# Attention with the new state ahead of the weighted values, and a last projection taken token tile by token tile

## What is computed

```python
# 1 gated linear attention, per batch and head, over time t
m_new = max(f + m, i); f_stab = exp(f + m - m_new); i_stab = exp(i - m_new)
C = f_stab * C + i_stab * outer(v, k);  n = f_stab * n + i_stab * k
y = sigmoid(o_gate) * (C @ q) / max(|n @ q|, 1)
# 2 MLP, 320 -> 2048 -> 320
h = x @ w_in;  x = maximum(0.01 * h, h) @ w_out
# 3 eight experts, 320 -> 1024 -> 320, weighted by P
P = exp(x @ w_gate), normed 8 times over rows and columns
out = sum over e of P[:, e] * (maximum(x @ w1[e], 0) @ w2[e])
```

## Time and profile before

| | us |
|---|---|
| median of 3 runs | 949.97 (949.3 to 950.03) |
| the profiled execution, its own time | 952.44 |
| its span, first to last instruction | 950.7 |
| TensorE busy in the span | 937.6 |
| mean granted TensorE clock | 0.996 |

### The profile page before, as it was taken

How to read it: one execution, slowest core, us unless ns; L and a number is a source line. 1 busy time by engine, 2 the same in 40 slices (tenths; PEclk the granted TensorE clock), 3 DMA queues, 4 the chain that set the end, 5 groups by cost and what they waited for, 6 DMA issues and landing times.

```text
span 950.7 us, 16706 instructions
## 1 busy us (share of the span) xinstructions
PE 937.6 (99%) x6529; PEld 892.7 (94%) x6529; DVE 648.5 (68%) x1066; ACT 360.6 (38%) x659; POOL 440.9 (46%) x501
## 2 busy tenths in 40 slices
PE   8999999999999999999999999999999999999998
PEld 5889888888789999999999999999999999999998
DVE  6577555457777899876766666676666666766664
ACT  5666443344454333333323332342343233233221
POOL 4364042046688656475742653473265257336000
PEclk9899999999999999999999999999999999999999
DMA  7961222002011111111211121021112101110000
GB/s 131 208 119 22 61 62 67 1 1 67 1 33 36 34 34 34 34 34 34 68 34 34 35 67 35 7 61 34 34 35 67 34 20 48 34 34 1 28 29 29
DMA packets 82796, 42.39 MB, mean 45 GB/s; under 512 B 54270, under 2 KB 82302, under 8 KB 82718
## 3 DMA queue, kind: packets, MB, share of 16 engines
q1 hardware_dynamic: 82510, 41.23, 17.0%
q10 hardware_dynamic: 208, 0.11, 0.0%
HBM read 39.13 MB, written 2.11 MB: 43 GB/s over the span
## 4 chain that ended last, share of the span: by engine, by line
PE 87%; DVE 6%; ACT 3%; issue 2%; DMA 1%; SPq 1%; POOL 0%; DVEq 0%; POOLq 0%; ACTq 0%
PE psB L1645 11%; PE psB L1647 11%; PE psB L1646 11%; PE psA L1631 8%; PE psA L1630 8%; PE psA L1629 8%; PE psA L1628 8%; PE psA L1558 7%; PE psB L1577 2%; PE psB L1579 2%; PE psB L1578 2%; PE psA L1456 2%; PE psB L1477 2%; DVE gl L1381 1%; PE psB L1584 1%
## 5 line engine op out<-in xcount | busy, mean ns | idle before, releaser
L677 POOL TENSOR_TENSOR wst<-raw_w,wst 128x128 fp32r<-128x128 f32 (+2 forms) x192 | 163.3, 863 | 303.9 <-ACT wst L896 175.1
L1645 PE MATMUL psB<-w2s,gh 128*128 128x320 f32 x768 | 238.6, 311 | 0.9 <-DVE acc L1355 0.9
L1647 PE MATMUL psB<-w2s,gl 128*128 128x320 f32 x768 | 237.3, 309 | 0.0
L1646 PE MATMUL psB<-w2s,gh 128*128 128x320 f32 x768 | 237.3, 309 | 0.0
L1003 ACT ACTIVATE gh<-part 128x512 fp32r<-128x512 f32 x192 | 110.9, 625 | 245.5 <-DVE part L1375 245.5
L1381 DVE SCALAR_TENSOR_TENSOR gl<-part,gh 128x512 fp32r<-128x512 f32 x192 | 160.5, 877 | 63.5 <-ACT gh L1003 62.9
L1631 PE MATMUL psA<-xop,wst 96*128 96x256 f32 x672 | 190.2, 283 | 0.0
L1630 PE MATMUL psA<-xop,wst 128*128 128x256 f32 x672 | 190.2, 283 | 0.0
L1629 PE MATMUL psA<-xop,wst 128*128 128x256 f32 x672 | 190.2, 283 | 0.0
L1628 PE MATMUL psA<-xop,wst 128*128 128x256 f32 x672 | 190.0, 283 | 0.0
L1645 PEld LDWEIGHTS psB<-w2s,gh 128*128 128x128 f32 x768 | 144.6, 188 | 1.3 <-DVE gl L1381 1.0
(11 more groups left out here) (196 smaller groups left out, 1393.1 us busy)
## 6 DMA issues: line engine op xcount, KB each, us to landing
raw_w<-in_moe_w_dram SPq DMA_DIRECT2D x32, 320.0 KB, 3.2
raw_w<-in_moe_w_dram SPq DMA_DIRECT2D x32, 256.0 KB, 2.6
raw_w<-in_moe_w_dram SPq DMA_DIRECT2D x96, 64.0 KB, 2.4
qs<-in_q_dram SPq DMA_DIRECT2D x12, 160.0 KB, 3.1
ks<-in_k_dram SPq DMA_DIRECT2D x12, 160.0 KB, 3.7
vz<-in_v_dram SPq DMA_DIRECT2D x12, 160.0 KB, 3.7
og<-in_o_gate_dram SPq DMA_DIRECT2D x12, 160.0 KB, 3.9
out_dram<-acc SPq DMA_DIRECT2D x5, 320.0 KB, 2.3
```

The lines of the kernel that those rows point to most:

```text
L677: return pool.tensor_tensor(dst, raw, high.bitcast(F32), ALU.subtract)
L1645: pe.matmul(bank, gh[:, slot, cols], w2[:, f, 0, :], start=first, stop=False)
L1646: pe.matmul(bank, gh[:, slot, cols], w2[:, f, 1, :], start=False, stop=False)
L1647: last = pe.matmul(bank, gl[:, slot, cols], w2[:, f, 0, :], start=False, stop=end)
```

## The change

In `pe_unit`, the new state of the unit before is taken ahead of its weighted values, where it stood behind the output transposes. Since d_done then no longer says that v has been read, `load_v` waits for y_prod as well. And after the last pair, `behind` does both halves of one token tile in each of its four parts; the first part waits for both halves of g.

```diff
             def load_v(n):
@@
                 at_least(sp, d_done, n - U_IT + 1)
+                at_least(sp, y_prod, n - U_IT + 1)
                 sp.dma_start(vz[j][:, :, 0:D], v[b, :, rows, :].rearrange("h s d -> s h d")).then_inc(v_in[j], 16)
@@
             def pe_unit(i, j, y=True):
                 transposes(i, j)
                 inter(i, j - 1)
+                new_state(i, j - 1)
                 intra(i, j - 1)
                 if y:
                     y_transposes(i, j - 2)
-                new_state(i, j - 1)
                 if 4 * i + j < NU - 1:
                     exponents(i, j + 1)
                 scores(i, j)
@@ def behind(n, k):
                     pe.wait_ge(y_read, (KT + 1) * (HALVES * NTB + 1))
+                if n == NP:
+                    if k == 0:
+                        pe.wait_ge(g2, 2 * m + 2)
+                    for f in (1, 0):
+                        expert_out(m, f, (k,))
+                    return
                 if k % 2 == 0:
                     pe.wait_ge(g2, 2 * m + 1 + k // 2)
                 expert_out(m, 1 if k < 2 else 0, (0, 1) if k % 2 == 0 else (2, 3))
```

## The result

The changed kernel takes 951.82 us (median of 21 executions, 951.3 to 953.3), the kernel before 949.90 (21 executions, 949.13 to 952.14): a ratio of 1.002 with a 95% interval of 1.0013 to 1.0027. It is slower by 1.9 us, where the forecast was 950.2 and no change that can be told. The time lies in the stated range of 948.4 to 954.5, but not near the forecast: the range had been drawn wide enough to reach into rival B, and that is where the time came out.

What follows compares the result with a forecast made beforehand. TensorE was taken to bound the kernel, so only its idle places and the tail could change. Attention rounds 0.0, last round +0.14 and last pair +0.06 gave +0.2 on the median 949.97: 950.2 us, range 948.4 to 954.5.

Steps and rivals of the forecast that it cites:

- rival B: Attention, the two sigmoid stops: the clock falls in the longer stops, at most 2.7 us per stop; slower; chance 0.31.
- Ordinary rounds: Attention rounds without a sigmoid: the moved new state fills the wait for ws, winning 0.24 us in each of five.
- the 0.14 by which I had it late: Attention, VectorE: ws starts about 0.14 us late after the reorder, still hidden by 0.22 in ordinary rounds.
- Sigmoid rounds: Two attention rounds bound by ScalarE's chain: 7.66 becomes 8.26 us, 0.60 longer each; stops about 2.0 us, from 1.0.
- Sum at full clock: Whole kernel: attention rounds 0.0, last round +0.14 and last pair +0.06, together +0.2 us.
- the last round: End of the attention: no new state covers the lateness of ws, costing +0.14 us.
- Early rounds: Attention before 35 us: no cost, since exponents wait for the third kt; bounds -0.6 and +0.6 us.
- Rival D: Start of the attention: moved matmuls fill an idle place at 23 us, escaping half clock; -2.7 us, 947.3; chance 0.05.
- rival C: Attention: ScalarE's chain has unseen slack, for instance if copies and casts give way; seven stops vanish, 948.5 us; chance 0.08.
- SP: Transfers on SP: load_v's added wait delays nothing, every transfer goes out no later than before; cost nothing.
- Last pair: End of the kernel: last read ends 0.07 us sooner, first weight load 0.13 later; together +0.06, bounds -0.2 and +0.3.
- the last transfer finding the others gone: Last store at the kernel's end: the favourable bound of the tail's estimate, -0.2 us.

Runs made afterwards that it cites:

- `before_fill`: Four matmuls of zeros added in round 2, ahead of the exponents of unit 3, to the kernel before; 949.74 us against 950.52, ratio 0.9994.
- the experiment on the last pair: The last pair's second projection done tile by tile, added alone to the kernel before; 950.08 us against 949.87, ratio 0.999.

## Where the prediction held and where it failed

**What bounds the kernel.** Held: from the first MLP matmul to the last gl are 848.8 us in the trace of after (94.38 to 943.20) and 848.7 in that of before (93.55 to 942.28), so only the attention and the last pair count, and in them the idle places of TensorE.

**Ordinary rounds.** The step that failed first: "the 0.60 fills the wait for ws; 0.24 is won". In the table an ordinary round falls by 0.24, to 6.26, only where it stands behind a stop for kt, with ScalarE's first x1 copy begun before TensorE's exponents (50.21 and 50.4 in the changed kernel's trace); in the three others it rises by 0.13, to 6.61. I had checked ws, wv, VectorE and the loads, and not what `transposes` itself waits for, exp_done. From the start of the output transposes ScalarE needed the same 2.78 us to the end of its exponentials in both kernels (43.05 to 44.81 + 1.02, and 41.77 to 43.53 + 1.02). TensorE, before, needed 3.18 from there to the next unit's transposes (43.05 to 46.23), and 0.60 of that was the new state. Without it TensorE would be there after 2.58, ahead of the exponentials; it went at 44.70, after 2.93. The 0.35 lost there is more than the 0.24 won at ws. The kernel with the casts moved shows it: 6.24 to 6.27 in every ordinary round. The three rounds are 1.1 us of the sum. ws stays hidden, as I had it, but not by my numbers: it starts 1.99 behind the scores' start in both kernels (44.55 less 42.56, 46.43 less 44.44), so the 0.14 by which I had it late did not come.

**Sigmoid rounds.** Held to the hundredth: 7.66 became 8.26, twice. The stop itself I put at about 2.0, and my own terms give 1.01 + 0.60 + 0.24 = 1.85; it measured 1.5, for 0.35 of the round's idle time now lies ahead of the transposes. With casts behind the exponentials, where the transposes don't wait, it is 1.85. That this gives back what the ordinary rounds win was right in sign; with the ordinary rounds above, the table's sum is +0.88 where the same rounds were put at about 0.

**Sum at full clock.** From the last exponents to the MLP's first matmul there are 0.09 more (8.35 with all stops filled, 8.26 in `before_fill`). I had +0.14 for the last round, with another cause: it is the wait for exponentials again, 0.35, less the 0.24 of ws. So the attention is +0.97, and with the last pair's -0.4 the sum is +0.5 to +0.6, where I had +0.2. That it is this near is luck: a term at 0.0 was +0.88, and one at +0.06 was -0.4.

**Clock.** Rival B, put at 0.31, is what decided. The changed kernel at a clock of 1.00 is 949.67 (measured with its early stop filled, since it never had 1.00 without) against 949.23 of before in the same set, +0.4; with all stops filled it is +0.7. The other 1.2 to 1.5 us of the result are clock that the changed kernel lost over what before loses. All 21 executions lost some (with the same attention and the old last pair, on another chip, nine of 12 did). How many of them lost it early and how many behind the later stops is not known, since only one of them was profiled; it lost about as much early as late. My reason for holding B the lesser case was that one fall is little to go by; the same rows already had the longer stops on the wrong side of the only fall seen. The busy time of those stretches came out at 2.5 of 4, not 2.0 to 2.1. My price of up to 2.7 for a stop was high, the half of it nearly right: a fall costs 1.6 here, since behind the second stop it was gone again at 82, with the end of the scores, and not after 6.8 us as early in the earlier trace rows. The rule of the Trainium skill that went with B (TensorE: Matmul & The Clock Gate, Part 1: bursts separated by waits can lose the full clock again) bears on this. The trace agrees in kind: 8 of 12 executions lost clock with the later stops idle, 0 of 12 with them filled.

**Early rounds.** Costed at nothing, bounds -0.6 and +0.6: measured in the table's first column -0.24, and the early fall about as frequent as it was (with the later stops filled, 6 of 12 executions lost clock, and of the kernel before 49 of 96). Rival D (the start escapes its half clock through the reorder) fell; rival C had the right idea that ScalarE's casts could give way, in the wrong place: they had to be moved.

**SP.** Held: the wait is empty.

**Last pair.** Put at +0.06 with bounds -0.2 and +0.3, measured -0.4, outside them. The first weight load was 0.24 behind its neighbour instead of 0.147, so 0.09 late where I had 0.13, and the reads ended as I had it within 0.1. The wrong term was the last store: I let it take as long as before. The last three stores now go 0.9 us apart instead of 0.5, and the two of 160 KB land in 1.8 us, not 2.3. The last one finds the DMA engines empty, where before they worked through all three without a pause (the rows under the experiment on the last pair). My bound for just this, the last transfer finding the others gone, was -0.2.

## What to carry to other kernels

When a group of instructions is moved, list what each of its neighbours waits for, not only the group itself: here the work was a cover for another engine's chain, and the wait that opened was of an instruction that the change did not touch. Follow the moved cover into the rounds with an exceptional long item (a table load, a sigmoid), for there the same move costs instead of winning; an order by round can have both. And compare executions by their granted clock: a stop lengthened by 0.5 us (its round by 0.6) cost 1.6 where the clock fell in it, more than its own length, and a few matmuls of zeros in the idle places brought that back.

## What the runs showed of the hardware

A stop of TensorE of 1.5 us, in 4 us of which it was busy for 2.5, took the clock to half in some executions and not in others (in one trace the second of two like stops, in another the first, in a third neither), and the scores behind it took 3.56 us for 1.95: such a fall is a step of 1.6 us in the time. Filling each of the two idle places with seven 128x512 bf16 matmuls of zeros (1.67 us), and the early one with four, kept 12 of 12 executions at full clock. And 160 KB stores issued 0.9 us behind the one ahead landed in 1.8 us, where they took 2.3 when issued 0.5 us behind.
